# Woven attention in a fused attention and two-layer FFN kernel: two slots per pair instead of four, and VectorE's scaling ahead of the maxima

## The reference

```python
# q, k, v: (batch 8, heads 8, seq 576, head_dim 64); chunks of 64 tokens, each attends to itself
scores = scale * np.matmul(q_c, k_c.transpose(0, 1, 2, 4, 3))
scores = scores - np.max(scores, axis=-1, keepdims=True)
attn = np.exp(scores)
attn = attn / (np.sum(attn, axis=-1, keepdims=True) + 1e-09)
out = np.matmul(attn, v_c)
x = out.transpose(0, 2, 1, 3).reshape(4608, 512)
# first FFN: w_gate, w_val (512, 1536), w_out (1536, 512)
rms = np.sqrt(np.mean(x * x, axis=-1, keepdims=True) + 1e-06)
xn = x / rms * rms_g
g = xn @ w_gate
y = (g / (1 + np.exp(-g)) * (xn @ w_val)) @ w_out
# second FFN: w_in2 (512, 2048), w_out2 (2048, 512)
h = y @ w_in2
return (h * np.clip(h + 3.0, 0.0, 6.0) / 6.0) @ w_out2
```

## Time and profile before

| | |
|---|---|
| three runs | 1674.45, 1676.81, 1678.32 us; median 1676.81 |
| profiled execution | span 1675.8 us (the profile gives no other time for it) |
| TensorE busy | 1645.6 us, 98% of the span |
| VectorE, ScalarE, GpSimd busy | 62%, 52%, 44% |
| mean granted TensorE clock | 0.995 of full speed |

### The profile page before, as it was taken

One profiled execution on the slowest core, in us unless ns is written; L12 is line 12 of the kernel. 1 busy time (PEld: TensorE's weight loads), 2 busy tenths in 40 slices (PEclk: granted clock), 3 DMA queues, 4 the chain that ended last, 5 costly groups with the idle time before them and its releaser, 6 DMA issues.

```text
span 1675.8 us, 31535 instructions
## 1 busy us (share of the span) xinstructions
PE 1645.6 (98%) x12297; PEld 1603.2 (96%) x12297; DVE 1034.0 (62%) x1407; ACT 867.4 (52%) x1375; POOL 731.0 (44%) x686
## 2 busy tenths in 40 slices
PE   7899999999999999999999999999999999999999
PEld 6788999999999999999999999999999999999999
DVE  4877868868755555664455776665666764444443
ACT  4665656655544444554444665554655653433432
POOL 2543434438786665432120467777766610010010
PEclk9999999999999999999999999999999999999999
DMA  9576767636465655888997866647648976676664
GB/s 177 133 186 150 172 164 177 151 118 192 152 231 203 206 206 184 315 311 306 313 317 287 300 228 235 223 178 254 221 162 300 377 252 199 200 224 204 197 222 132
DMA packets 334692, 366.98 MB, mean 219 GB/s; under 512 B 185104, under 2 KB 300560, under 8 KB 331344
## 3 DMA queue, kind: packets, MB, share of 16 engines
q1 hardware_dynamic: 322976, 334.69, 63.1%
q0 software_dynamic: 7104, 28.84, 4.8%
q10 hardware_dynamic: 4464, 1.44, 0.5%
HBM read 200.80 MB, written 164.10 MB: 218 GB/s over the span
## 4 chain that ended last, share of the span: by engine, by line
PE 85%; DVE 3%; DMA 3%; issue 3%; POOL 3%; SPq 2%; ACT 2%; DVEq 0%; ACTq 0%; POOLq 0%
PE bx L934 13%; PE by L934 12%; PE bx L936 12%; PE bx L935 12%; PE by L936 12%; PE by L935 12%; PE att L936 2%; PE att L934 2%; PE att L935 2%; PE att L900 2%; PE att L858 1%; DMA hl_b<-h_scratch 1%; SPq L539 1%; PE att L909 1%; PE att L881 1%
## 5 line engine op out<-in xcount | busy, mean ns | idle before, releaser
L934 PE MATMUL bx<-tx,wr 128*128 128x384 f32 x840 | 288.2, 343 | 2.7 <-ACT gb L1130 2.0
L934 PE MATMUL by<-tx,wr 128*128 128x384 f32 x840 | 287.3, 342 | 0.8 <-DVE ub L1479 0.6
L936 PE MATMUL bx<-tx,wr 128*128 128x384 f32 x840 | 281.9, 336 | 0.0
L935 PE MATMUL bx<-tx,wr 128*128 128x384 f32 x840 | 281.8, 335 | 0.0
L936 PE MATMUL by<-tx,wr 128*128 128x384 f32 x840 | 281.6, 335 | 0.0
L935 PE MATMUL by<-tx,wr 128*128 128x384 f32 x840 | 281.4, 335 | 0.0
L1505 DVE TENSOR_TENSOR hl_d<-hl_d 128x1536 fp32r<-128x1536 f32 x84 | 147.8, 1790 | 121.1 <-ACT hl_d L1210 121.0
L1505 DVE TENSOR_TENSOR hl_b<-hl_b 128x1152 fp32r<-128x1152 f32 x84 | 115.7, 1389 | 113.1 <-ACT hl_b L1210 112.5
L1210 ACT ACTIVATE hl_d<-hl_d 128x1536 fp32r<-128x1536 f32 x84 | 122.7, 1483 | 98.8 <-DMA hl_d<-u_scratch 98.5
L934 PEld LDWEIGHTS bx<-tx,wr 128*128 128x128 f32 x840 | 158.5, 189 | 7.0 <-issue 3.5
L934 PEld LDWEIGHTS by<-tx,wr 128*128 128x128 f32 x840 | 158.0, 188 | 4.9 <-DVE ub L1479 1.8
(11 more groups left out here) (184 smaller groups left out, 4365.0 us busy)
## 6 DMA issues: line engine op xcount, KB each, us to landing
hl_d<-u_scratch SPq DMA_DIRECT2D x84, 768.0 KB, 4.6
hl_b<-h_scratch SPq DMA_DIRECT2D x84, 576.0 KB, 6.2
u_scratch<-ut SPq DMA_DIRECT2D x48, 576.0 KB, 3.7
h_scratch<-ht SPq DMA_DIRECT2D x36, 576.0 KB, 3.6
u_scratch<-ub SPq DMA_DIRECT2D x96, 192.0 KB, 3.1
u_scratch<-ub SPq DMA_DIRECT2D x48, 384.0 KB, 2.5
h_scratch<-vb SPq DMA_DIRECT2D x72, 192.0 KB, 3.4
h_scratch<-vb SPq DMA_DIRECT2D x36, 384.0 KB, 3.1
```

The source lines that it names most:

```text
L934: pe.matmul(dst, w_hi, m_hi, start=start, stop=False, skip_group_check=not opens)
L935: pe.matmul(dst, w_hi, m_lo, start=False, stop=False, skip_group_check=not opens)
L936: return pe.matmul(dst, w_lo, m_hi, start=False, stop=stop, skip_group_check=not opens)
```

## The change

The numbers in `EARLY` and `AFTER` and the offsets in `at_slot_of` change, and VectorE's scale_attention stands ahead of transpose_qk and shift_scores within a slot. Attend(n) now shares a slot with scores(n + 1), and xT(n) one with probsT(n + 1), for all woven units but the first and the last. Before, the 30 units used 109 slots, nine of them with two pieces; now they use 60, 58 of them with two.

```diff
     S_FIRST = NG
-    EARLY = {6: (-6, -3, 1, 7), 7: (0, 3, 8, 12), 8: (7, 9, 14, 20), 9: (12, 15, 21, 24), 10: (18, 23, 26, 31), 11: (24, 28, 33, 37), 12: (32, 37, 39, 44), 13: (38, 43, 48, 51), 14: (46, 49, 52, 58), 15: (51, 53, 59, 64), 16: (57, 61, 66, 73), 17: (64, 66, 75, 77)}
-    AFTER = {7: 5, 8: 1, 11: 5, 12: 5, 14: 1, 16: 5, 17: 5}
+    EARLY = {6: (-6, -3, 1, 6), 7: (1, 6, 8, 12), 8: (8, 12, 14, 19), 9: (14, 19, 21, 25), 10: (21, 25, 27, 31), 11: (27, 31, 33, 37), 12: (33, 37, 39, 44), 13: (39, 44, 46, 50), 14: (46, 50, 52, 56), 15: (52, 56, 58, 62), 16: (58, 62, 64, 68), 17: (64, 68, 70, 75)}
+    AFTER = {7: 5, 8: 1, 14: 1}
     SC, TR, AT, XX = 0, 1, 2, 3
 
     def at_slot_of(n, piece):
-        return EARLY[n][piece] if n in EARLY else 7 * n - 53 - min(3, (n - 12) // 2) + (0, 5, 8, 13)[piece]
+        return EARLY[n][piece] if n in EARLY else 7 * n - 53 - min(3, (n - 12) // 2) + (0, 5, 7, 12)[piece]
...
                 if m > 0 and slot == 1:
                     gated(m - 1, H11)
+                n = woven(m, slot, AT, 1)
+                if n is not None:
+                    scale_attention(n)
                 n = woven(m, slot, SC, 1)
                 if n is not None and n + 1 < NN and next_transposed_after(n) == 1:
                     transpose_qk(n + 1)
                 if n is not None:
                     shift_scores(n)
-                n = woven(m, slot, AT, 1)
-                if n is not None:
-                    scale_attention(n)
```

## The result

| | before | after |
|---|---|---|
| median | 1677.57 us (1674.45 to 1679.13, 4 runs) | 1705.56 us (1701.88 to 1706.18, 4 runs) |
| ratio, 95% interval | | 1.0156 [1.0131, 1.0181] |
| span of the profiled execution | 1675.8 us | 1704.4 us |
| mean granted TensorE clock | 0.995 | 0.988 |

The change makes the kernel 28 us slower. The forecast was 1683.2 us, 6.4 more than before, with a range up to 1689: the sign is right, the size is more than four times too small.

What follows compares the result with a forecast made beforehand. Early, SyncE's queue behind transpose_qk(11) sets the pace; from 140 to 380 us only TensorE's own work counts. Early +7.6 and late -1.2 make +6.4 us on 1676.8: 1683.2 us, range 1674.5 to 1689.

Steps and rivals of the forecast that it cites:

- late part: From xT(12) to xT(35): pairs save 2.2 us, four-slot units cost 1, steady units nothing; together -1.2 us.
- Early part: From attend(6) to xT(12): t0 later by 7.0 us and the last leg by 0.6, together +7.6 us.
- steps 1 and 2: From slot 6: xT(6) waits until about 65.0, then low clock; transpose_qk(9) ends about 73.2, attend(8) starts about 82.9.
- Step 3: From attend(8) to the end of transpose_qk(11): 16.3 us, giving 99.2 instead of 92.2, 7.0 us later (5 to 9).
- t0: End of transpose_qk(11), after which SyncE's queue was said to set the pace; 92.2 us before, forecast 99.2.
- Step 4: SyncE's queue behind t0: attend(10) idles 5 us, attend(11) waits until t0 + 21, xT(12) at t0 + 41.5, 0.6 later.
- four-slot units: Units 13 to 16, where attend to xT is four slots: 1 us in total (0 to 4).
- By its own sign: The late step counts as wrong if TensorE idles over 2 us between xT(12) and 380 us.
- The pairs: probsT with xT saves nothing; attend with scores saves 0.10 us (0 to 0.21), 22 pairs, 2.2 us (0 to 4.6).
- the queue bites harder: Rival: waits at attend(8), attend(10), attend(11) each lower the clock, and four-slot units wait; +11.6 us, 1688.4 us, chance 0.18.
- It cancels: Rival: clock stays up after slot 6 or SyncE's run shortens, and pairs save 3.3 us; 1677.0 us, chance 0.18.
- faster: Rival: t0 does not move and pairs save both entry and exit, 4.6 us; 1672.2 us, chance 0.14.

Runs made afterwards that it cites:

- the two halves: The change's slots for units 6 to 13 alone, before's from 14 on: 1695.34 us; before's slots to 13, the change's from 14 on: 1684.86 us.
- the kernel with the chosen pairs: Before's slots to unit 18, pairs from 19 except units 19, 25, 31, normalisation a slot earlier from 19, the change's VectorE order: 1678.62 us, ratio 1.0007 against before.

## Why the prediction was wrong in size

In places of the span, as the prediction counts: xT(12) came 13.6 us later where +7.6 was forecast, the late part took 9.4 more where -1.2 was, and what is behind 5.5 more where nothing was. The three misses, 6.0, 10.6 and 5.5, are the 22 us between the 6.4 forecast and the 28.6 of the two spans.

**Early part, steps 1 and 2: right.** xT(6) waited until 64.61 (forecast about 65.0), the granted clock was 0.66 from 64 to 72, transpose_qk(9) ended at 72.9 (73.2), attend(8) came at 82.67 (82.9).

**Step 3, t0: too small.** I put 16.3 us from attend(8) to t0; it took 102.6 - 82.7 = 19.9. The reason stands in the step itself as a case that I did not take: the wait at attend(8) brings the clock down a second time, to 0.66 in the window 82 to 92, which is 3.4 us of work; xT(8) waits another 0.68 us. I had already read in the earlier trace rows that such a wait is followed by a low clock, and then counted it for one wait of three. So t0 moved by 10.4, not 7.0.

**Step 4: the queue right, the last leg wrong.** The queue kept its times (attend(10) idle for 5.72, forecast 5; v(12) issued at t0 + 26.6, forecast about 27), and the two kernels that moved t0 alone show that xT(12) goes with it: +3.6 for +3.2, -0.6 for -1.0. But the idle time ahead of attend(11) did not come (it started at t0 + 22.1, its v loads were issued at t0 + 16.7), and xT(12) came at t0 + 44.1, not 41.5. I had put "GpSimd's sums and xT(12) follow" the x store. The sums did: GpSimd waited 0.65 us for the store, not 3.65, and unit 12's inverse rms was ready at t0 + 38.7. What held xT(12) then was ScalarE's program, with the exponential and two more table loads inside the silu. No kernel moved that exponential alone, so its price is read from the trace only.

**Late part: the failed step.** "I cost the steady units 18 to 35 at nothing, covered by VectorE's and ScalarE's free quarter" and 1 us for the four-slot units: -1.2 in all with the pairs. Measured +9.4, or +10.5 for equal work. Both terms were too small. From xT(12) to xT(18), which holds the four-slot units, the change lost 5.5 us (6.6 for equal work) where 1 us (0 to 4) less the pairs' gain was put; from xT(18) to xT(35) it lost 3.9, where the pairs alone should have gained. In the steady units the waits that the trace lists come at three of them, 19, 25 and 31, in steps in which ScalarE also fills operands (L1105). A free quarter of an engine's time is no cover where its program is in a fixed order: the mean square stands behind a snapshot that waits for a product, and the normalisation behind two more. The kernels with the earlier normalisation show it: same slots, same work, 8.9 us less in the late part. I had written down the price if the cover was gone, "up to one slot" a unit, and left it out of both the sum and the range. TensorE has 8.3 us of waits from xT(12) to xT(35) in the profile after (0.5 before): 3.9 at units 13 to 16 and 4.4 at units 19, 25 and 31, with 5.7 us withheld by the clock (1.7 before). By its own sign, over 2 us idle there, the late step was wrong.

**The pairs.** probsT with xT saves nothing, as forecast. Attend with scores saves 0.20 to 0.22, the upper bound, not the 0.10 that I took: no drain remains inside the pair that the trace could show (attend to scores 0.98 us, scores to the product 0.98). The Trainium skill, "TensorEngine Tiling (Array Packing)", section Tiling Modes, says that a change of tiling mode drains the engine; I had read from it that half the gain would stay lost inside the pair, and these rows show no such price: each block takes the 0.98 us that it takes alone. With 22 pairs this would be 2.4 us more than forecast, and all of it was lost to waits.

**The rivals.** The one that came nearest is "the queue bites harder": the waits at attend(8) and attend(10) did bring the clock down, the one at attend(11) did not come. Its 1688.4 was still 17 us short, since it did not have the late part. "It cancels" and "faster" both needed a t0 that stays; it did not.

**Open.** The 5.5 us behind the weave (4.5 for equal work), in code that did not change. They are there in both profiles of the change and in the kernel with the loads moved (+4.6), but not in the two halves (0.0 and 0.0), and four kernels are 2 to 3 us better there than before. Most of it lies in the second FFN's up products: 356.7 us in the profile after, 352.4 before, and 350.3 to 350.8 in six of the other kernels. In the profile after, seven products behind 420 us wait 0.3 us each for a combine (L1479, 2.0 us in all), in before two. What sets them off isn't shown. It was also not tried whether an early table with pairs exists that leaves t0 in its place.

## What to carry to other kernels

Cost a step that gives an engine's chain fewer slots by the order of that engine's program: find what stands ahead of each link and what that waits for. A share of free time says nothing about it. Where the trace before shows a low clock behind a wait of TensorE, count each new wait of that length twice, once for itself and once for the clock behind it, and carry that into the next step of the chain. When a piece moves by one slot, look also at what it now parts: an exponential inside a silu cost ScalarE two more table loads. And where one queue sets the pace, find the one event that lets it start, and price the change by how far it moves that event.

## What the runs showed of the hardware

- The low clock behind a wait cost nearly as much as the waits themselves (12 to 13 us of work not done in the weave, beside 16.6 us more of idle time). With each of three waits of 3.3, 3.6 and 5.7 us went 6.8 us at the lower level of 1.2 GHz, begun in the wait or just behind it; what of this lay behind the wait cost 2.4, 3.4 and 2.6 us of work. Short waits can do it too: after the 1.13 us at 180.41 and the 0.71 us ahead of xT(15) the window from 180 to 190 shows 0.83, after the 1.59 us at 217.94 the one from 218 to 228. But the 1.10 us ahead of xT(14), and the 1.25 us ahead of xT(25) in the kernel with the chosen pairs, left the clock at 1.00: one such wait alone need not.
- Work that nothing needs, put into three waits, kept the granted clock at 1.00 from 62 to 72 us and from 110 to 120 (0.66 in the change), and gave 5.7 us back in the weave.
- ScalarE's change between the exponential and the silu is a table load of 1.28 us each time.
- Two blocks of sixteen small matmuls each (64x65, then 64x64) follow each other with no gap: 0.98 us from start to start, and the entry and exit are paid once.
